# Sink-row products, an opening's marks and a batch of biases placed anew in a fused attention and mixture kernel

## The chip, the cores and the metric

The kernel runs on one core of one Trainium2 chip. The metric is the device time of one execution in microseconds (us). Engines are named PE (TensorE, with PEld for its weight loads), DVE (VectorE), ACT (ScalarE), POOL (GpSimd) and SP (SyncE, which only issues DMAs here).

## The reference, cut to what matters

```python
# 1 attention: batch 4, heads 8, sequence 768, head size 64, n_sink 4, window 128
scores = scale * q @ k.T
keep = (pos_k < n_sink) | ((0 <= pos_q - pos_k) & (pos_q - pos_k < window))
a = exp(where(keep, scores, -1e9) - max);  a /= a.sum(-1) + 1e-9
x = (a @ v) as rows of 512                       # 3072 tokens
# 2 mixture of 8 experts, one expert a token
logits = x @ w_gate + modality_bias[modality_id]
e = argmax(logits);  gate = softmax(logits)[e]
out[e == k] = gate * (relu(x @ w1[k]) @ w2[k])   # 512 -> 1024 -> 512
# 3 dense layer
h = out @ w_in;  g = h * sigmoid(1.702 * h);  return g @ w_out   # 512 -> 2048 -> 512
```

## The kernel before, in words

All three stages lie in one program. Float32 operands of the large products are split into a rounded high part and a low part, and products are added from the parts.

**Attention steps.** Attention runs as 192 steps, 48 for each batch b (step n within it): six query tiles (i = n mod 6) for each of 8 heads. I number them all through as k = 48b + n. In step k PE makes the scores of tile k (L950, L951), turns the probabilities of tile k-3 (`turn_probs`, L964, at i = 5 of that tile also the sink columns, L968) and weighs V with those of tile k-4 (`weigh_values`, L989, L996). DVE masks the scores and finds their minimum (L1802), ACT takes the exponential (L1371), ACT moves turned probabilities out of PSUM (L1406), DVE does so for the sixth tile of a head (L1814, L1815, L1818). Every engine has the same written order, and semaphores bind them: the scores of tile k want the mask of tile k-3 done, for they use three PSUM banks.

**Pairs of heads.** A pair g is two heads, 12 steps. For each pair PE multiplies V transposed by the gate weights and takes the sink rows of V (`weigh_gates`, in two parts, L1016 x6 each and L1022 x2), DVE moves the first (`move_gates`, L1847) and splits the second into a high and a rest (`split_sinks`, L1857, L1859), and ACT lays the split rows out in four blocks (`lay_sinks`, L1398). `ahead(k, at)` says for which pair something falls due in step k. V transposed comes by `load_vt` (L465), issued by SP after it has stored a finished pair (L477) and before it loads further Q, K and V. These loads wait on buffers to come free.

**GpSimd.** POOL splits Q and K of heads 1 to 31 (`split_qk`: L663, L664, L666, L669), and after some heads it does other pieces of work by the dictionary `between`. Head h cannot be scored before its split.

**The opening.** One expert is chosen from batch 0's tokens and two tiles of it are computed while the rest is sorted. POOL adds biases (`open_logits`), marks ties (`open_ties`), counts (`open_chain`, L719), chooses (`open_choice`), makes six one-hot marks (`open_marks`, the marks at L748). DVE does the reductions in between, at fixed steps (`choose_open`, `index_open`), and PE ranks (`rank_open`, step 29 of batch 1) and sorts (`sort_open`, step 17 of batch 2). ACT rounds that expert's weights in 16 pieces at steps given by `cast_at` (L1438), POOL makes their rest in `split_open`.

**The early routing.** The first 18 tiles are routed before attention ends. After its last split POOL adds biases (L788), DVE takes the maximum (L1778, step 34 of batch 3), POOL marks ties (L791 to L795), issues two gathers (`gather_open`, L774) and counts, ending at L817, which sets `tiles_seen`. PE's `rank_early` (L1033) waits for that in step 46 of batch 3 (k = 190), before it turns and weighs.

**After attention** come the opening's products (L1109), the tables and gathers, the runs over experts, and the dense layer.

## Time and profile before

| what | value |
|---|---|
| time, median of 3 runs | 1090.27 us (1090.04 to 1091.02) |
| the profiled execution's own time | 1090.47 us |
| its span, first to last instruction | 1088.7 us |
| mean granted TensorE clock | 0.998 of full |
| busy: PE, PEld, DVE, ACT, POOL | 1077.4, 922.8, 441.6, 405.2, 342.1 us |
| attention, from the first scores to the opening's first product | 10.36 to 222.96 us |

The span leaves 1.8 us of the profiled execution outside of it. A busy PE is a modelled one: ends of matmuls overlap the next ones, so the time of a step is read from start to start, and idle time from the brackets of the timeline. POOL's row in the page is full up to about 217 us and nearly empty afterwards; PE's is full from 10 us to the end.

### The profile page before, as it was taken

The page shows a single profiled execution, that of the slowest core. Times are in us where ns is not written, and L with a number is a line of the kernel's source. Part 1 is how long each engine was busy: PE and PEld are TensorE (multiplying, and loading weights), DVE is VectorE, ACT ScalarE, POOL GpSimd, SP SyncE. Part 2 cuts the span into 40 slices and gives each one's busy share as a digit, 9 for nine tenths or more (in the row PEclk, how much of TensorE's full clock was granted, in tenths as well). Part 3 has the DMA queues.
Part 4 walks back from the last instruction along what each step waited for, and adds up shares of the span by engine and source line. Part 5 has one row for each costly group of instructions (what it writes and reads, how often), then busy time and mean ns, then how long its engine had stood idle before and what let it go on. Part 6 is the DMA issues. An engine that isn't in the chain of part 4 may idle for free.

```text
span 1088.7 us, 18538 instructions
## 1 busy us (share of the span) xinstructions
PE 1077.4 (99%) x5819; PEld 922.8 (85%) x5820; DVE 441.6 (41%) x1137; ACT 405.2 (37%) x863; POOL 342.1 (31%) x425
## 2 busy tenths in 40 slices
PE   9999999999999999999999999999999999999998
PEld 8999999888788888888888888888888888888887
DVE  6777767797122252222463232223323323223222
ACT  5777778743222242222352222222222222222222
POOL 8999999844266221211130010001001001000000
PEclk9999999999999999999999999999999999999999
DMA  9977888253811133121231001001001101000001
GB/s 235 223 178 190 225 222 234 70 176 111 280 41 39 55 129 112 39 87 39 99 116 47 20 20 31 27 0 48 19 10 39 29 10 39 0 0 9 30 1 39
DMA packets 59186, 90.23 MB, mean 83 GB/s; under 512 B 7936, under 2 KB 32512, under 8 KB 59136
## 3 DMA queue, kind: packets, MB, share of 16 engines
q1 hardware_dynamic: 53376, 70.72, 23.5%
q0 software_dynamic: 5760, 18.89, 5.0%
q8 instruction: 25, 0.41, 0.2%
q14 instruction: 25, 0.20, 0.1%
HBM read 70.18 MB, written 19.41 MB: 82 GB/s over the span
## 4 chain that ended last, share of the span: by engine, by line
PE 84%; POOL 9%; DVE 2%; DMA 2%; issue 2%; ACT 1%; POOLq 0%; DVEq 0%; ACTq 0%
PE psum L1295 8%; PE psum L1297 8%; PE psum L1296 8%; PE psum L1288 8%; PE psum L1286 8%; PE psum L1287 8%; PE psum L1226 4%; PE psum L1232 4%; PE psum L1229 4%; PE psum L1195 4%; PE psum L1199 4%; PE psum L989 4%; PE psum L1203 4%; POOL k_lo L669 2%; POOL q_st L666 2%; PE psum L964 2%
## 5 line engine op out<-in xcount | busy, mean ns | idle before, releaser
L2099 DVE TENSOR_TENSOR g<-psum,g 128x512 f32<-128x512 f32 x96 | 66.3, 691 | 292.2 <-ACT g L1535 292.2
L1535 ACT ACTIVATE g<-psum 128x512 f32<-128x512 f32 x96 | 57.4, 599 | 305.3 <-PE psum L1288 304.5
L1295 PE MATMUL psum<-w_hi,gT_hi 128*128 128x512 f32 x384 | 151.3, 394 | 0.0
L1297 PE MATMUL psum<-w_hi,gT_lo 128*128 128x512 f32 x384 | 149.6, 390 | 0.0
L1296 PE MATMUL psum<-w_lo,gT_hi 128*128 128x512 f32 x384 | 149.6, 389 | 0.0
L1288 PE MATMUL psum<-x2T,win_lo 128*128 (+1 forms) x384 | 149.5, 389 | 0.0
L1286 PE MATMUL psum<-x2T,win_hi 128*128 (+1 forms) x384 | 149.5, 389 | 0.0
L1287 PE MATMUL psum<-x2T,win_hi 128*128 (+1 forms) x384 | 149.4, 389 | 0.0
L919 POOL DMA_INDIRECT out<-o_out,out_rows x20 | 21.5, 1076 | 406.2 <-ACT o_out L1555 401.6
L989 PE MATMUL psum<-v_sb,pT 128*128 128x74 f32 x704 | 105.9, 269 | 3.9 <-ACT pT L1406 0.9
L989 PEld LDWEIGHTS psum<-v_sb,pT 128*128 128x128 f32 x704 | 93.9, 192 | 11.4 <-DVE pT L1815 6.5
L1802 DVE CUSTOM_DVE_ANT_0 s_msk<-psum,mask_sb 128x260 f32<-128x260 f32 (+1 forms) x192 | 76.4, 403 | 56.4 <-PE psum L951 39.0
L1371 ACT ACTIVATE probs<-s_msk,negmax 128x260 f32<-128x260 f32 (+1 forms) x192 | 92.7, 494 | 12.2 <-issue 8.3
L2106 DVE TENSOR_TENSOR gT_lo<-g,gT_hi 128x512 fp32r<-128x512 f32 x96 | 66.5, 693 | 64.5 <-ACT gT_hi L1542 64.5
L1542 ACT CAST gT_hi<-g 128x512 fp32r<-128x512 f32 x96 | 59.6, 621 | 74.6 <-DVE g L2099 74.6
L1297 PEld LDWEIGHTS psum<-w_hi,gT_lo 128*128 128x128 f32 x384 | 72.1, 188 | 15.2
L1287 PEld LDWEIGHTS psum<-x2T,win_hi 128*128 128x128 f32 x384 | 72.1, 188 | 15.0
L1288 PEld LDWEIGHTS psum<-x2T,win_lo 128*128 128x128 f32 x384 | 72.1, 188 | 15.0
L1286 PEld LDWEIGHTS psum<-x2T,win_hi 128*128 128x128 f32 x384 | 72.1, 188 | 14.9
L1296 PEld LDWEIGHTS psum<-w_lo,gT_hi 128*128 128x128 f32 x384 | 72.2, 188 | 14.4
L1295 PEld LDWEIGHTS psum<-w_hi,gT_hi 128*128 128x128 f32 x384 | 72.1, 188 | 14.3
L1486 ACT CAST hT_hi<-psum 128x512 fp32r<-128x512 f32 x52 | 28.1, 590 | 120.1 <-PE psum L1214 120.1
(315 smaller groups left out, 1912.8 us busy)
## 6 DMA issues: line engine op xcount, KB each, us to landing
qk_raw<-qkT SPq DMA_DIRECT2D x32, 390.0 KB, 6.3
stage<-w SPq DMA_DIRECT2D x12, 1024.0 KB, 8.6
qk_raw<-qkT SPq DMA_DIRECT2D x32, 198.0 KB, 6.8
x<-y_rows SPq DMA_DIRECT2D x24, 256.5 KB, 2.6
vT_sb<-vT SPq DMA_DIRECT2D x16, 384.0 KB, 4.9
v_sb<-vP SPq DMA_DIRECT2D x16, 384.0 KB, 6.6
x_rows<-x_sb SPq DMA_DIRECT2D x16, 384.0 KB, 3.4
win_raw<-w SPq DMA_DIRECT2D x16, 256.0 KB, 4.5
```

Source lines behind the costliest of these rows:

```text
L989: mm = pe.matmul(o, pT[:, n % 2, k * P:(k + 1) * P], v_sb[:, c, kb, half * VEXT:(half + 1) * VEXT], start=(i == 0 and k == 0), stop=(k == ...
L1286: pe.matmul(bank, wh, hi, start=(c == 0), stop=False)
L1287: pe.matmul(bank, wh, lo, start=False, stop=False)
L1288: mm = pe.matmul(bank, win_lo[:, c, f * P:(f + 1) * P], hi, start=False, stop=(c == CH - 1))
L1295: pe.matmul(psum[:, OB[t], :], gh, hi, start=(f == 0), stop=False)
L1296: pe.matmul(psum[:, OB[t], :], gh, lo, start=False, stop=False)
L1297: return pe.matmul(psum[:, OB[t], :], gT_lo[:, f % 4, t * P:(t + 1) * P], hi, start=False, stop=(f == F2C - 1))
L1371: act.activation(probs[:, n % RING, 0:width[i]], s_msk[:, n % RING, 0:width[i]], ACT.Exp, bias=negmax[:, n % 8:n % 8 + 1], scale=-1.0).the ...
L1542: act.copy(gT_hi[:, f % 4, :], g32[:, f % 2, :]).then_inc(gT_high, 1)
L1802: dve.tensor_tensor_reduce(s_msk[:, n % RING, 0:width[i]], psum[:, S_ps[n % 3], 0:width[i]], mask_sb[:, min(i, MASKS - 1), 0:width[i]], -S ...
L2099: dve.tensor_tensor(g32[:, f % 2, :], psum[:, FB[f % 2], :], g32[:, f % 2, :], ALU.mult)\
L2106: dve.tensor_tensor(gT_lo[:, f % 4, :], g32[:, f % 2, :], gT_hi[:, f % 4, :].bitcast(F32), ALU.subtract).then_inc(gT_split, 1)
```

## The change

The gate products and sink rows of pair g move: pair 0 stays, pair 1 stays, and pair g from 2 on starts in step 3 of pair g-1, where it started in step 9. Spreading is in the same step, the move two steps later, the split three and four later, the laying of one block a step from five to eight later. The six one-hot marks go from POOL to DVE, which compares with an iota row that PE has put into PSUM. POOL's `open_choice` comes after head 15 and no longer 16. The early biases and tie marks, which followed POOL's last split, follow heads 27 and 29. Several of DVE's small steps and PE's two opening products have other step numbers. SP loads V transposed of pair 2 before it loads V of pair 1.

```diff
-    VW_AT, VW_LEAD = 1, 9
+    VW_AT, VW_NEXT, VW_LEAD = 1, 9, 3
-    OPEN_RANK_STEP, OPEN_INV_STEP = 29, 17
+    OPEN_RANK_STEP, OPEN_INV_STEP = 33, 20
+    IOTA_AT = 256
     def ahead(k, at):
-        first, later = k - VW_AT - at, k % (2 * QT) - VW_LEAD - at
-        if first == 0:
-            return 0
-        return k // (2 * QT) + 1 if later == 0 and k // (2 * QT) + 1 < B * PAIRS else None
+        for g in range(B * PAIRS):
+            begin = VW_AT if g == 0 else VW_NEXT if g == 1 else (g - 1) * (2 * QT) + VW_LEAD
+            if k == begin + at:
+                return g
+        return None
...
# SP
             for h in range(SLOT + 1, H):
+                if h == SLOT + 1:
+                    load_vt(2)
                 load_v(0, h - SLOT)
                 sp.wait_ge(qk_split, SPLITS * (h - SLOT))
                 load_qk(0, h)
-                if h == SLOT + 1:
-                    load_vt(2)
...
# GpSimd, open_marks
-                then(pool.tensor_tensor(o_place[:], o_place[:], o_row[:], ALU.add))
+                pool.tensor_tensor(o_place[:], o_place[:], o_row[:], ALU.add).then_inc(open_placed, 1)
...
-                for t in range(QT):
-                    pool.tensor_scalar(open_oh[:, t, :], iota_row[:], o_place[:, t:t + 1], None, ALU.is_equal)\
-                        .then_inc(open_marked, 1)
+                pool.sem_inc(open_placed, 1)
...
+            def add_biases():
+                pool.wait_ge(logits_added, B - 1)
+                pool.tensor_tensor(lg[:, 0:PRE, :], lg[:, 0:PRE, :], bias_of[:, 0:PRE, :], ALU.add).then_inc(biased, 1)
+            def mark_ties():
+                pool.wait_ge(best_found, 1)
...             # the same three operations that stood after the loop
-            between = {2: make_iotas, 5: make_consts, 9: make_biases, 11: open_logits, 12: open_ties, 13: open_chain, 16: open_choice,
-                       18: open_marks, 25: open_rows}
+            between = {2: make_iotas, 5: make_consts, 9: make_biases, 11: open_logits, 12: open_ties, 13: open_chain, 15: open_choice,
+                       18: open_marks, 25: open_rows, 27: add_biases, 29: mark_ties}
...
# PE, weigh_gates
-                    if g == PAIRS + OPEN_RANK_STEP // (2 * QT) + 1:
-                        pe.wait_ge(open_keyed, 1)
                     if g == 2 * PAIRS + OPEN_INV_STEP // (2 * QT) + 1:
-                        pe.wait_ge(open_indexed, 1)
+                        pe.wait_ge(open_marked, QT)
# PE, rank_open
-                pe.wait_ge(vw_moved, 2 * (PAIRS + OPEN_RANK_STEP // (2 * QT) + 1))
-                pe.wait_ge(sinks_split, PAIRS + OPEN_RANK_STEP // (2 * QT) + 1)
+                pe.wait_ge(sinks_split, PAIRS + OPEN_RANK_STEP // (2 * QT) + 2)
...
+                pe.wait_ge(consts_made, 6)
+                pe.matmul(psum[:, VW_ps, IOTA_AT:IOTA_AT + P], ident[:], iota_row[:], start=True, stop=True)
# PE, sort_open
-                pe.wait_ge(vw_moved, 2 * (2 * PAIRS + OPEN_INV_STEP // (2 * QT) + 1))
-                pe.wait_ge(sinks_split, 2 * PAIRS + OPEN_INV_STEP // (2 * QT) + 1)
+                pe.wait_ge(sinks_split, 2 * PAIRS + OPEN_INV_STEP // (2 * QT) + 2)
+                pe.wait_ge(open_placed, 2)
...
# ACT
-                if n < HT and g == 0 and at in (6, 7):
-                    lay_sinks(g, (2 * at - 12, 2 * at - 11))
-                elif n < HT and g and at in (2, 3):
-                    lay_sinks(g, (2 * at - 4, 2 * at - 3))
-                if b == 1 and n == 3 * QT + 2:
+                for t in range(SINK_T):
+                    g = ahead(b * HT + n, 5 + t)
+                    if n < HT and g:
+                        lay_sinks(g, (t,))
+                    if n < HT and g == 0 and t < SINK_T // 2:
+                        lay_sinks(g, (2 * t, 2 * t + 1))
+                if b == 1 and n == 27:
                     act.wait_ge(open_shifted, 1)
...
# DVE, choose_open (batch 1): o_best 12 -> 13, o_lead 18 -> 24, o_gate 22, 23, 24 -> 37, 39, 41,
#   ranks OPEN_RANK_STEP + 1 -> + 2, o_most + 2 -> + 3
-                if n == 18:
+                if n == 24:
                     dve.wait_ge(open_tied, 1)
                     dve.tensor_reduce(o_lead[:], o_tied[:], AX.X, ALU.max).then_inc(open_lead, 1)
...
# DVE, index_open (batch 2)
+                if n in (9, 11, 12):
+                    t = 2 * (9, 11, 12).index(n)
+                    if t == 0:
+                        dve.wait_ge(open_placed, 1)
+                    for t in (t, t + 1):
+                        dve.tensor_scalar(open_oh[:, t, :], psum[:, VW_ps, IOTA_AT:IOTA_AT + P], o_place[:, t:t + 1], None,
+                                          ALU.is_equal).then_inc(open_marked, 1)
-                if n == OPEN_INV_STEP + 2:
+                if n == OPEN_INV_STEP + 3:
...
# DVE, route_early (batch 3)
-                if n == 34:
-                    dve.wait_ge(pre_biased, 1)
+                if n == 25:
+                    dve.wait_ge(biased, 2)
                     dve.tensor_reduce(best[:, pre], lg[:, pre, :], AX.X, ALU.max).then_inc(best_found, 1)
-                if n == 37:
+                if n == 36:
                     dve.wait_ge(ties_marked, 1)
...
-                if n == 44:
+                if n == 45:
                     add_heads(B - 1, H - 2)
# DVE, step
-                if n < HT and at in ((4, 5) if g == 0 else (0, 1)):
-                    split_sinks(g, at % 4)
+                for k in range(2):
+                    if n < HT and ahead(b * HT + n, 3 + k) is not None:
+                        split_sinks(ahead(b * HT + n, 3 + k), k)
```

## Rows read from the trace of the kernel before

**Rows 1.** Busy time by stretch: us, PE, PEld, DVE, ACT, POOL, clock, DMA, GB/s

```profile
74.49:87.20 12.71, 12.59 (x110) 12.26 (x110) 9.24 (x45) 9.90 (x31) 12.13 (x14) 1.00 0.73 186
...
125.58:139.87 14.29, 13.36 (x117) 12.93 (x116) 9.39 (x47) 10.85 (x32) 13.81 (x11) 1.00 0.89 218
139.87:152.82 12.95, 12.75 (x110) 12.25 (x110) 9.07 (x43) 10.70 (x32) 12.63 (x11) 1.00 0.87 219
...
191.90:205.07 13.17, 12.97 (x110) 12.29 (x110) 8.84 (x42) 10.60 (x32) 12.77 (x10) 1.00 0.25 71
205.07:218.21 13.14, 11.64 (x90) 10.19 (x90) 9.29 (x42) 9.96 (x29) 9.07 (x20) 1.00 0.26 71
```

**Rows 2.** Groups of POOL's instructions: count, busy us, mean ns, idle before

```profile
L669 POOL TENSOR_TENSOR k_lo<-qk_raw,k_hi 128x792 fp32r<-128x792 f32 x31 | 58.1, 1874 | 2.4
```

**Rows 3.** The chain that ended last, in order of time: start, us

```profile
120.97 3.51 POOL open_oh L748 x6
...
206.89 0.07 DVE best L1778
```

**Rows 4.** Timeline of POOL: start, us, instruction, idle before

```profile
86.53 0.27 POOL L719 TENSOR_TENSOR o_tied<-o_tied,o_lead 128x48 f32<-128x48 f32 x1
...
124.43 0.82 POOL L663 CAST q_st<-qk_raw 64x768 fp32r<-64x768 f32 x1
...
207.27 0.43 POOL L791 TENSOR_TENSOR below<-lg,best 128x144 f32<-128x144 f32 x1 [0.42 <-DVE best L1778]
...
209.52 1.23 POOL L774 DMA_INDIRECT open_xs<-x_rows,open_gather  x1 [0.57 <-issue]
...
216.39 0.19 POOL L817 CAST seen<-batch_sum 128x8 fp32r<-128x8 f32 x1
```

**Rows 5.** Timeline of PE: start, us, instruction, idle before

```profile
39.44 0.27 PE L964 MATMUL psum<-ident,probs 128*128 128x128 f32 x1
...
49.04 0.31 PE L950 MATMUL psum<-k_hi,q_st 128*128 128x128 f32 x1
...
87.20 0.31 PE L950 MATMUL psum<-k_hi,q_st 128*128 128x128 f32 x1
...
136.01 0.81 PE L1016 MATMUL psum<-sink_w,vT_sb 128*128 128x16 f32 x6 [0.81 <-issue]
...
145.46 0.67 PE L989 MATMUL psum<-v_sb,pT 128*128 128x74 f32 x4
...
217.66 0.23 PE L1033 MATMUL psum<-onehot,tri 128*128 128x144 f32 x1
```

**Rows 6.** Timeline of DVE, the same columns

```profile
49.69 0.29 DVE L1802 CUSTOM_DVE_ANT_0 s_msk<-psum,mask_sb 128x128 f32<-128x128 f32 x1 [0.21 <-ACT probs L1371]
...
49.90 0.36 DVE L1857 TENSOR_SCALAR v_sinks_hi<-psum,signs 128x144 fp32r<-128x144 f32 x1
...
81.36 0.20 DVE L1731 TENSOR_REDUCE o_lead<-o_tied 128x6 f32<-128x48 f32 x1
...
206.89 0.30 DVE L1778 TENSOR_REDUCE best<-lg 128x18 f32<-128x144 f32 x1 [2.08 <-POOL lg L788]
```

**Rows 7.** Timeline of ACT, the same columns

```profile
143.15 0.62 ACT L1438 CAST win_hi<-win_raw 128x512 fp32r<-128x512 f32 x1
...
144.37 0.64 ACT L1398 CAST v_sinks<-v_sinks_all 32x144 fp32r<-32x144 f32 x2
```

**Rows 8.** SP's issue of V transposed for pair 3, and its landing

```profile
35.40 1.57 SPq L465 DMA_DIRECT2D vT_sb<-vT  x1
...
DMA to landing us min/median/max: 4.5/4.5/4.5
```

**Rows 9.** Where the clock fell: one stretch, and PE's timeline in and after it

```profile
246.00:260.00 14.00, 13.98 (x71) 12.01 (x72) 11.02 (x26) 6.23 (x8) 3.28 (x2) 0.88 0.13 39
...
249.21 2.05 PE L1128 MATMUL psum<-win_hi,hT_hi 128*128 128x512 f32 x4
...
259.34 1.18 PE L1128 MATMUL psum<-win_hi,hT_hi 128*128 128x512 f32 x4
```

More of the change, by code:

```diff
@@ L378, in program @@
         spare_known = sem("spare_known")
-        logits_added, pre_biased, best_found = sem("logits_added"), sem("pre_biased"), sem("best_found")
+        logits_added, biased, best_found = sem("logits_added"), sem("biased"), sem("best_found")
         ties_marked, lead_found = sem("ties_marked"), sem("lead_found")
         expert_known, consts_copied = sem("expert_known"), sem("consts_copied")
-        open_biased, open_best, open_shifted, open_tied = (sem(f"open_{k}") for k in ("biased", "best", "shifted", "tied"))
+        open_best, open_shifted, open_tied = (sem(f"open_{k}") for k in ("best", "shifted", "tied"))
         open_lead, open_exped, open_gated, open_seen = (sem(f"open_{k}") for k in ("lead", "exped", "gated", "seen"))
         open_ranked, open_keyed, open_chosen = (sem(f"open_{k}") for k in ("ranked", "keyed", "chosen"))
-        open_expert_known, open_marked, open_inverted = (sem(f"open_{k}") for k in ("expert_known", "marked", "inverted"))
+        open_expert_known, open_placed, open_marked = (sem(f"open_{k}") for k in ("expert_known", "placed", "marked"))
+        open_inverted = sem("open_inverted")
         open_indexed, open_high, open_split, open_low = (sem(f"open_{k}") for k in ("indexed", "high", "split", "low"))
@@ L776, in gather_open @@
                         .then_inc(open_gathered[t], 16)
-            between = {2: make_iotas, 5: make_consts, 9: make_biases, 11: open_logits, 12: open_ties, 13: open_chain, 16: open_choice,
-                       18: open_marks, 25: open_rows}
+            def add_biases():
[3 more added lines that the diff above has]
+                pool.wait_ge(best_found, 1)
+                pool.tensor_tensor(below[:, 0:PRE, :], lg[:, 0:PRE, :], col(best[:, 0:PRE], some), ALU.subtract)\
+                    .then_inc(shifted, 1)
+                pool.wait_ge(shifted, 1)
+                then(pool.tensor_scalar(tied[:, 0:PRE, :], below[:, 0:PRE, :], 0.0, None, ALU.is_equal))
+                pool.tensor_tensor(tied[:, 0:PRE, :], tied[:, 0:PRE, :],
+                                   from_end[:].rearrange("p (o e) -> p o e", o=1).broadcast_to(some), ALU.mult)\
+                    .then_inc(ties_marked, 1)
+            between = {2: make_iotas, 5: make_consts, 9: make_biases, 11: open_logits, 12: open_ties, 13: open_chain, 15: open_choice,
+                       18: open_marks, 25: open_rows, 27: add_biases, 29: mark_ties}
             for h in range(1, B * H):
@@ L785, in _ @@
                     split_open(h - OPEN_BACK)
-            pool.wait_ge(logits_added, B - 1)
-            pool.tensor_tensor(lg[:, 0:PRE, :], lg[:, 0:PRE, :], bias_of[:, 0:PRE, :], ALU.add).then_inc(pre_biased, 1)
-            pool.wait_ge(best_found, 1)
-            pool.tensor_tensor(below[:, 0:PRE, :], lg[:, 0:PRE, :], col(best[:, 0:PRE], some), ALU.subtract)\
-                .then_inc(shifted, 1)
-            pool.wait_ge(shifted, 1)
-            then(pool.tensor_scalar(tied[:, 0:PRE, :], below[:, 0:PRE, :], 0.0, None, ALU.is_equal))
-            pool.tensor_tensor(tied[:, 0:PRE, :], tied[:, 0:PRE, :],
-                               from_end[:].rearrange("p (o e) -> p o e", o=1).broadcast_to(some), ALU.mult)\
-                .then_inc(ties_marked, 1)
             gather_open()
@@ L1725, in choose_open @@
                 counts = psum[:, VW_ps, OPEN_RANK + QT * E:OPEN_RANK + (QT + 1) * E]
[L1726 to L1727 removed]
+                if n == 13:
+                    dve.wait_ge(biased, 1)
                     dve.tensor_reduce(o_best[:], o_lg[:], AX.X, ALU.max).then_inc(open_best, 1)
[L1729 removed]
+                if n == 24:
                     dve.wait_ge(open_tied, 1)
                     dve.tensor_reduce(o_lead[:], o_tied[:], AX.X, ALU.max).then_inc(open_lead, 1)
[L1732 removed]
+                if n == 37:
                     dve.wait_ge(open_exped, 1)
                     then(dve.tensor_reduce(o_gate[:], o_exps[:], AX.X, ALU.add))
[L1735 removed]
+                if n == 39:
                     then(dve.tensor_scalar(o_gate[:], o_gate[:], 1e-9, None, ALU.add))
[L1737 removed]
+                if n == 41:
                     dve.reciprocal(o_gate[:], o_gate[:]).then_inc(open_gated, 1)
[L1739 removed]
+                if n == OPEN_RANK_STEP + 2:
                     dve.wait_ge(open_ranked, 1)
```

15 lines of the change are left out of this document (3 added, 12 removed).

## The prediction

> **What bounds the kernel now.** I read the page first: PE is full from 10 us to the end, POOL up to 217 us, so all that this edit touches lies in attention. The chain of waits then shows who leads there. From 120.97 us on, POOL's marks and its splits stand in it, up to DVE's maximum at 206.89 [rows 3]; the reader should not take this for a PE that waits on splits. POOL is never short of work: 31 splits of 5.4 us each, of which one of four instructions is shown, have 2.4 us of idle before them in all [rows 2]. But PE starts each head 2 to 7 us after its split. What makes the chain run along POOL is that its early biases stand behind the last split, and DVE stops 2.08 us for them in step 34 [rows 6], which stops PE.
>
> Stretches of one pair, from scores to scores, give PE's own pace: 12.71 us where nothing disturbs [rows 1]. Above that I find: 1.58 us in 125.58:139.87; 0.24 in 139.87:152.82 and likewise in the two pairs behind it; 0.46 in 191.90:205.07 and in the pair ahead of it; and 205.07:218.21, which is the last pair's first eleven steps. Those should take 12.71 less one step (0.9) and less the gate products that it does without (1.5), 10.3, and take 13.14 [rows 1].
>
> The point that decides is the last wait. PE's ranking product starts at 217.66 [rows 5]; it needs POOL's last count, which ends at 216.39 + 0.19 = 216.58 [rows 4]. PE reaches that place only 1.1 us after POOL is ready. So of what PE gains, only 1.1 us count before POOL must gain as well. The end of attention, the opening's products and the long rest hang on this point, and I carry a shift of it unchanged to the end.
>
> **PE's side, part by part.**
> - Gate products of pair g from step 9 to step 3. PE's count of work is the same. In a head without them PE waits in its fourth step for DVE's move of the sixth tile (some 0.3 us); the products cover that wait. Covered heads and bare heads change places, 14 for 14. Nothing.
> - The old wait for the index. Products of pair 10 (k = 117) waited for DVE: 0.81 us idle [rows 5], 1.05 in the step. They now lie at k = 111 and wait only for marks that DVE ends in k = 108. Gain 1.05. The remaining 0.53 of the 1.58 is the sort, which moves to k = 116 and stays.
> - ACT. In even heads two blocks, one rounded weight piece (0.62) and two more blocks (0.64 for two) pile up [rows 7], and PE's product at 145.46 [rows 5] comes 0.24 late. With one block a step in the odd head the heap is 1.24 us by the step that was late, where it was 1.9. I take all of it as gone: 6 x 0.24 + 3 x 0.21 = 2.1, with 0 as the other end.
> - DVE's stop for the biases. Of the 2.8 us that the last stretch has above its pace, 0.2 are the ranking and 0.45 ACT's heap; 2.1 are left, as long as DVE's wait of 2.08 [rows 6]. I take 1.9, for PE may run on a little. Gone, for POOL adds them after head 27, at about 181 us, and DVE asks at k = 169, about 191.
> - The ranking of the opening moves from k = 77, where it cost 0.2, to the bare fourth step of k = 81, where PE would wait anyway; the added iota product (0.2 by the spacing of two 128-column products) goes there too. Gain 0.2 to a loss of 0.2; I take 0.1.
> - Six marks on DVE. No row has this form from PSUM. Nearest: a 128x144 scaling out of PSUM takes 0.36 [rows 6]; so at most 6 x 0.36 = 2.2 us in three steps, at least 0 for PE, as DVE has 0.8 us idle in the fourth step and 0.4 in the sixth. I take 0.2.
> - V transposed of pair 3. This is a new wait. It was wanted at k = 33, about 45 us; now at k = 27. It is issued at 35.40 and lands 4.5 later, at 39.9 [rows 8], and SP cannot be earlier, as its queue is jammed by the store ahead. PE comes to k = 27's products at 39.44 [rows 5], where ahead of that it turned probabilities. So PE stands 0.5 us. For other pairs the load lands 2 us or more ahead. Bounds: 0, and 1.5 if the earlier stores shift. ACT's spreading waits with it, 0.3 us of work that PE's second part does not miss. The swap of pair 2's load and pair 1's V on SP costs nothing: both land by about 24, wanted at 26 and 28.
>
> Sum for PE: 1.05 + 2.1 + 1.9 + 0.1 - 0.2 - 0.5 = 4.4; it would come to the ranking at about 213.2.
>
> **POOL's side.** Its last count at 216.58 shifts by:
> - marks removed: from 120.97 [rows 3] to 124.43 [rows 4], -3.46.
> - a new wait after head 13. `open_chain` starts at 86.53 [rows 4], and now DVE gives the lead in k = 72, not in k = 66. PE starts k = 72 at 87.20 [rows 5]. Mask follows scores by 0.65 (49.04 [rows 5] to 49.69 [rows 6]), the next operation starts 0.21 behind, and the reduction takes 0.20 (81.36) [rows 6]: 87.20 + 0.65 + 0.21 + 0.20 = 88.26, with 0.1 for the semaphore 88.35. That is 1.8, and as PE is 0.5 late by pair 3's load, 2.3. Behind the waiting instruction stand the splits of heads 14 on; those have 3 us and more to spare, so PE misses nothing, but every later piece of POOL is late by it. Lower end 1.8, upper 3.3.
> - choice after head 15: POOL is there at 102.6, DVE's key is ready at 101.3. No wait.
> - biases and ties moved ahead of the last splits. Before, from 206.37, the end of the last split, to the gathers at 209.52 [rows 4] it is 3.15 us, 0.42 of it the wait for the maximum. After: biases 0.43 and ties 1.63 among splits, and 0.61 from the last split to the gathers: 2.67. So -0.48. The splits of heads 30 and 31 end at about 201.9 and 207.3; PE wants them at 202.5 and 208.5.
>
> Sum: -3.46 + 2.3 - 0.48 = -1.6. The last count ends at 216.58 - 1.6 = 215.0, PE ranks at 215.1, 1.9 us after it came there. The kernel is 217.66 - 215.1 = 2.6 us shorter. Behind the wait PE's products stand close, so I give nothing back there.
>
> Span 1088.7 - 2.6 = 1086.1; the profiled execution 1090.47 - 2.6 = 1087.9. That execution lies 0.2 above the median of 1090.27, which gives 1087.7. All that PE gains beyond POOL is lost in that wait; so even if ACT's heap stays (2.1), the time barely moves.
>
> **Rivals.**
> - PE is the bound (chance 0.13). If POOL's new wait is absent or its counting has slack, PE comes at 213.2: 4.4 shorter, 1085.9; if pair 3's load does not stop it, 1085.4. For it speaks that the range of both sums overlaps within a microsecond or so; against it, that DVE cannot give the lead before scores of k = 72 exist.
> - No change to be measured (0.17). POOL waits longer, by 2 us more in all: 1088.5 to 1090.3. A PE that is late in any step up to k = 72 passes its lateness to POOL one for one, so a load of pair 3 that lands at 41.5 would do the most of it. For: SP's issue of that load took 1.57 us, where others take 0.5. Against: SP's order from 16 us on is the same as before.
> - The clock (0.10). PE's new stop of 1.9 us comes in a stretch of small products. In the old trace the clock is 0.88 over 246 to 260 [rows 9], that is, at 1.2 GHz for a part and 2.4 for the rest, after small transposes and 64-column products; four 512-column products took 2.05 instead of 1.18 there [rows 9], and with the next four 1.5 us were lost. The stops of 0.5 to 0.8 us in attention cost no clock. If the new one does, 1.5 us are given back: 1089.2. [...]
> - Slower (0.10). The bare fourth step. If the products in step 3 do not cover the even head's wait while the odd head's is bared, and ACT's rounding with blocks in the same steps adds its 0.24, PE loses 0.3 + 0.24 in each of 14 pairs, 7.6 us, against gains of 4.4: PE ranks at 220.8, 3.1 later, 1093.4. It decides from 0.3 us a pair on, and can be told from 0.5. Against it: DVE does the same in-head steps in both heads, and old odd heads with products show no wait.
>
> **Chances and range.** The forecast, 1086.9 to 1088.8, has 0.50. A tell-tale difference from no change is 0.2%, 2.2 us, so faster begins below 1088.1: two thirds or so of the forecast and all of the first rival make 0.48, and same is 0.42; slower 0.10. For eight in ten I take 1085.3 to 1090.5, which holds all but the slow case and some of the tails.
>
> **What would show it.** In the changed trace: POOL idle about 2.3 us before L719's successor, on DVE's lead; PE idle about 0.5 us at pair 3's products near 39.5 and about 1.9 us before the ranking near 213; no idle at k = 117; DVE's maximum with no wait; pairs of 12.7 us from 140 to 200. If PE is not idle before the ranking, POOL is not the bound, and the second sum holds. Wrong would be the forecast if a pair's pace is no longer 12.71, or if the long rest behind 223 us does not shift as one piece.

## The result and the profile after

The changed kernel takes 1099.01 us, the median of 6 runs (1097.22 to 1103.53), beside 1090.28 (1090.04 to 1091.54) for the kernel before: a ratio of 1.0089, 95% interval 1.0075 to 1.0103. It is 8.7 us slower. The forecast was 1087.7 us, with 0.10 for slower.

The profiled execution took 1097.22 us, its span 1095.5. PE's first scores start at 9.96 us in it (10.36 before). Two marks carry the comparison: POOL's last count, and PE's ranking product, which follows it. From the timeline of the changed kernel (start us, us, engine, line):

```profile
224.35 0.19 POOL L822 CAST seen<-batch_sum 128x8 fp32r<-128x8 f32 x1
...
226.65 0.23 PE L1036 MATMUL psum<-onehot,tri 128*128 128x144 f32 x1
```

Before, the count ended at 216.58 [rows 4] and PE ranked at 217.66 [rows 5]. So the ranking is 9.0 us later, and it comes 2.1 us after the count is done: PE, not POOL, is late. At the end of the span 6.7 of the 9.0 are left. Most of the difference is a part of 246 to 260 us that the old profiled execution had at 1.2 GHz (it cost 1.5 us, by the spacing of PE's products there); the same window of the changed kernel has a granted clock of 1.00. Stretches from scores to scores, in the columns of [rows 1]:

```profile
63.58:77.89 14.31, 13.32 (x110) 12.36 (x110) 9.87 (x44) 10.00 (x30) 13.76 (x12) 1.00 0.71 174
77.89:91.37 13.48, 13.13 (x111) 12.37 (x110) 9.24 (x44) 9.98 (x30) 8.40 (x9) 1.00 0.69 175
132.98:147.20 14.22, 13.95 (x117) 13.07 (x116) 10.16 (x47) 11.02 (x32) 13.82 (x13) 1.00 0.80 202
147.20:160.68 13.48, 13.12 (x111) 12.35 (x110) 9.41 (x47) 11.03 (x32) 13.16 (x11) 1.00 0.81 211
202.02:215.59 13.57, 13.21 (x110) 12.36 (x110) 9.26 (x44) 10.88 (x32) 10.37 (x11) 1.00 0.23 70
215.59:227.21 11.62, 11.21 (x91) 10.13 (x90) 8.86 (x40) 9.56 (x28) 7.50 (x16) 1.00 0.26 80
```

The reader should see three things. An undisturbed pair takes 13.48 us and not 12.71 [rows 1], with the same count of instructions on PE (111 and 110 in the stretch) and a full clock: PE waits. The pair at the start of a batch takes 14.31 (three of them do, k = 48, 96 and 144). And what the change meant to remove did go: the last stretch, to PE's ranking step, takes 11.62 where it was 13.14.

Who is waited for stands in the view of waits (us in total, times, longest). The changed kernel:

```profile
PEld psum L994 <- ACT pT L1410: 12.7, 35, 0.8
POOL o_tied L721 <- DVE o_lead L1736: 5.8, 1, 5.8
POOL below L786 <- DVE best L1789: 5.1, 1, 5.1
```

and the same wait of PE's weight loads in the kernel before:

```profile
PEld psum L989 <- ACT pT L1406: 3.8, 11, 0.8
```

POOL's two waits of 5.8 and 5.1 us look like the culprit in such a list. They are not: PE's ranking does not follow POOL by the shortest step, as the first fence shows. The new waits are PE's on ACT's move of turned probabilities, 35 where there were 11. The timeline of PE shows their spacing at the start of an even head, by the first score product (L955) of k = 84, 85 and 86 in the changed kernel:

```profile
91.37 0.31 PE L955 MATMUL psum<-k_hi,q_st 128*128 128x128 f32 x1
...
92.64 0.37 PE L955 MATMUL psum<-k_hi,q_st 128*128 128x260 f32 x1
...
93.90 0.36 PE L955 MATMUL psum<-k_hi,q_st 128*128 128x260 f32 x1
```

Each of these steps takes 1.27 us, where they take 0.86 and 0.91 before. And ACT in that stretch, where it lays the blocks that stand in steps k = 82 and 83 of its written order:

```profile
91.41 0.31 ACT L1402 CAST v_sinks<-v_sinks_all 32x144 fp32r<-32x144 f32 x1
91.74 0.37 ACT L1410 COPY pT<-psum 128x256 f32<-128x256 f32 x1
92.14 0.51 ACT L1375 ACTIVATE probs<-s_msk,negmax 128x260 f32<-128x260 f32 x1
92.68 0.31 ACT L1402 CAST v_sinks<-v_sinks_all 32x144 fp32r<-32x144 f32 x1
93.01 0.37 ACT L1410 COPY pT<-psum 128x256 f32<-128x256 f32 x1
```

From move to move it is 1.27 us (91.74 to 93.01), ACT never idle: move, exponential and one block, one behind the other. The kernel before, where no block lay between, in the timeline of ACT:

```profile
79.41 0.37 ACT L1406 COPY pT<-psum 128x256 f32<-128x256 f32 x1
79.81 0.51 ACT L1371 ACTIVATE probs<-s_msk,negmax 128x260 f32<-128x260 f32 x1
80.23 0.35 ACT L1406 COPY pT<-psum 128x256 f32<-128x256 f32 x1
80.48 0.51 ACT L1371 ACTIVATE probs<-s_msk,negmax 128x260 f32<-128x260 f32 x1
81.00 0.37 ACT L1406 COPY pT<-psum 128x256 f32<-128x256 f32 x1
```

There a move starts before the exponential ahead of it has ended (80.23 against 79.81 + 0.51), and from move to move it is 0.77 to 0.82 us. A block of 0.31 us thus lengthens this chain by 0.45 or more, and the step of PE beside it has only 0.1 us to spare.

The batch starts have a second cause. VectorE's timeline at n = 6 and 7 of batch 2 (k = 102 and 103) in the changed kernel:

```profile
127.53 0.36 DVE L1868 TENSOR_SCALAR v_sinks_hi<-psum,signs 128x144 fp32r<-128x144 f32 x1
127.92 0.84 DVE L1665 TENSOR_REDUCE lg<-lg_parts 128x48 f32<-128x384 f32 x1
129.09 0.43 DVE L1813 CUSTOM_DVE_ANT_0 s_msk<-psum,mask_sb 128x260 f32<-128x260 f32 x1 [0.33 <-ACT probs L1375]
```

The sum over the heads of the batch before (`add_heads` at n = 6) now stands behind the first half of V's split, which used to lie elsewhere in a pair, and the mask of k = 103 starts at 129.09, 1.5 us behind PE's scores of that step (127.54). PE pays for it two steps on: k = 57, 105 and 153 take 1.96 to 1.98 us instead of 1.41. That is 0.55 of the 0.83 us that such a pair takes above 13.48; the other 0.29 lie at k = 50, 98 and 146 (1.36 us, where the same step of a later pair takes 1.07). At k = 50 and 146 most of them go when ACT's blocks are placed otherwise (1.05 to 1.12 us in the runs below).

### The profile page after: what moved, and what is told of

It reads as the page before. It is cut to its first block, busy times and chain, and to the rows that moved or that the text cites. A ratio compares the mean times of both kernels' runs of the same rounds, so it can differ in the third digit from the quotient of the medians.

```text
span 1095.5 us, 18568 instructions
## 1 busy us (share of the span) xinstructions
PE 1081.7 (99%) x5821; PEld 922.4 (84%) x5822; DVE 444.1 (41%) x1143; ACT 407.8 (37%) x863; POOL 340.4 (31%) x419
## 4 chain that ended last, share of the span: by engine, by line
PE 89%; ACT 4%; issue 2%; DVE 2%; DMA 2%; POOL 1%; POOLq 0%; DVEq 0%; ACTq 0%
PE psum L1299 8%; PE psum L1301 8%; PE psum L1300 8%; PE psum L1292 8%; PE psum L1290 8%; PE psum L1291 8%; PE psum L994 5%; PE psum L1230 4%; PE psum L1236 4%; PE psum L1233 4%; PE psum L1199 4%; PE psum L1203 3%; PE psum L1207 3%; PE psum L969 2%; PE psum L1218 2%
## 5 line engine op out<-in xcount | busy, mean ns | idle before, releaser
L994 PE MATMUL psum<-v_sb,pT 128*128 128x74 f32 x704 | 109.0, 274 | 8.2 <-DVE pT L1826 2.6
```

The lines of the kernel that those rows point to most:

```text
L994: mm = pe.matmul(o, pT[:, n % 2, k * P:(k + 1) * P], v_sb[:, c, kb, half * VEXT:(half + 1) * VEXT], start=(i == 0 and k == 0), stop=(k == ...
```

## The experiments

All comparisons are with runs of the kernel before made beside them. To set profiled executions side by side I use the distance from PE's first scores to its ranking: 207.3 us before (217.66 - 10.36) and 216.7 after (226.65 - 9.96), so 9.4 us is what has to be explained. Where a profiled execution has a stretch at half clock inside that distance, I take out what its steps took above the same steps of a neighbouring kernel, and say so.

**Two blocks a step in the quiet steps.**

```diff
-                for t in range(SINK_T):
-                    g = ahead(b * HT + n, 5 + t)
-                    if n < HT and g:
-                        lay_sinks(g, (t,))
+                for t in range(SINK_T // 2):
+                    g = ahead(b * HT + n, 5 + t)
+                    if n < HT and g is not None:
+                        lay_sinks(g, (2 * t, 2 * t + 1))
```

> The changed kernel with one thing put back: ScalarE lays two blocks a step, in the third and fourth step of the odd head (k = 8, 9 mod 12), not one a step in k = 8 to 11. Theory (ScalarE is the bound in a pair since a block lies in steps 4 and 5 of a head, where it also moves probabilities in every step): a pair of batch 1 or 2 goes from 13.48 back to 12.7 us, 14 to 15 pairs give 11 us back at PE's ranking (226.65 to about 215.5), and the kernel takes 1087 to 1090 instead of 1099.0. Rival (the gate products in the even head's fourth step, or V's split on VectorE in steps 6 and 7, slow the pair): the pair stays at 13.3 us or more, the time at 1097 or more. Each pair that crosses the start of a batch keeps its extra 0.8 us by both.

Measured: 1091.16 us (12 runs), before 1091.19 (29), ratio 1.0012 (0.9995 to 1.0030). A pair, in the view of stretches of this kernel:

```profile
50.70:63.42 12.72, 12.60 (x110) 12.27 (x110) 9.04 (x42) 9.87 (x31) 12.05 (x13) 1.00 0.80 199
```

The ranking comes 209.4 us after the first scores, 207.2 without the 2.3 us that k = 9 to 12 took too long in this one execution: 0.7 in k = 9, where PE stood for the load of pair 1's V transposed (landed at 19.75 us, in the other profiled kernels between 17.6 and 18.4), the rest at half clock from 22.4 us on. That is 9.5 us less than 216.7, all of the 9.4, and the main theory holds: ACT's blocks are the loss. I had put the time at 1087 to 1090, and the median came out 1.2 us above; part of what was missing is in the later pairs, where two blocks and a rounded weight piece share a step (k = 83 and 107 take 1.40 us, not 0.95, and k = 131 and 143 take 1.26).

**One block a step, in quiet steps only.** The four blocks at k = 8, 9, 14 and 15 mod 12:

```diff
+                for t, late in enumerate((5, 6, 11, 12)):
+                    g = ahead(b * HT + n, late)
+                    if n < HT and g is not None and g > 1:
+                        lay_sinks(g, (t,))
```

> The changed kernel with one block a step, but only in ScalarE's two quiet steps of each head: k = 8, 9, 14, 15 mod 12 instead of 8 to 11. Theory (it is the place of a block, not the number in a step): as with two blocks a step in k = 8 and 9, a pair of 12.7 us and 1087 to 1090 us, within 1 us of that kernel. Rival (one block a step is slow by itself, as each starts ScalarE's chain anew): a pair between 12.9 and 13.5, over 1092.

Measured: 1088.99 us (12 runs), before 1091.19, ratio 0.9983 (0.9967 to 0.9998). The undisturbed pairs fall to 12.65 us, under the 12.71 of the kernel before (pairs 0 and 1 keep two blocks a step). The ranking comes 210.05 us after the first scores, 204.9 without the 5.1 us that k = 27 to 32 took too long (see pair 3 below), 11.7 less than in the changed kernel:

```profile
79.13:91.78 12.65, 12.53 (x110) 12.26 (x110) 9.25 (x44) 9.99 (x31) 7.78 (x8) 1.00 0.73 187
```

One block a step is no harm in itself; the place is.

**The blocks alone, in the kernel before.**

```diff
-                elif n < HT and g and at in (2, 3):
-                    lay_sinks(g, (2 * at - 4, 2 * at - 3))
+                elif n < HT and g and at in (2, 3, 4, 5):
+                    lay_sinks(g, (at - 2,))
```

> The kernel before with one thing of the change: blocks of V's sink rows are laid one a step, in k = 2, 3, 4, 5 mod 12 of the even head, not two a step in k = 2 and 3. All else, gate products and splits too, stays. Theory (a block in steps 4 and 5 makes ScalarE the bound): 0.6 to 0.8 us more a pair, 15 pairs, so 9 to 12 us: 1099 to 1102. Rival (the loss of the change needs the moved products or splits): within 2 us of 1090.3.

Measured: 1098.43 us (6 runs), before 1091.19, ratio 1.0072 (1.0055 to 1.0090). The ranking is 216.6 us after the first scores, 9.3 later than before. Its pairs:

```profile
77.74:91.21 13.47, 13.11 (x110) 12.33 (x110) 9.23 (x45) 10.14 (x31) 12.12 (x20) 1.00 0.72 183
```

One edit of the change, alone, gives its undisturbed pair of 13.47 to 13.48 us and as large a loss at the ranking. The sums agree partly by chance: each of the two kernels has losses and gains of its own in single steps (here k = 75 takes 2.56 us instead of 1.42, and the stop for the biases at k = 181 to 183, 1.75 us, is hidden). The moved gate products are not needed for the slow pair, and with ACT's blocks out of the way they do not slow it either (12.72 and 12.65 us above).

**Half the dose.** One block in the last two steps of a head, where the change has two:

```diff
+                for late, blocks_of in ((5, (0, 1)), (6, (2,)), (7, (3,))):
+                    g = ahead(b * HT + n, late)
+                    if n < HT and g:
+                        lay_sinks(g, blocks_of)
```

> The changed kernel with blocks at k = 8 (two), 9 (one) and 10 (one) mod 12: one block in the head's last two steps, where there were two. Theory (ScalarE has no room in these steps, so each block there is lateness in full and is worked off in the next head's first steps): half of the loss, 0.4 us a pair: a pair of 13.1 us, PE's ranking 211.9 us after its first scores (207.1 with both blocks out of these steps, 216.7 with both in them), time 1093 to 1094.5. Rival (there is a point beyond which the pair tips over): a pair of 12.7 or of 13.5 us, the time within 1.5 us of one of the two.

Measured: 1093.83 us (5 runs), before 1089.19 (17 runs), ratio 1.0042 (1.0026 to 1.0057); the ranking 210.5 us after the first scores, 1.4 less than I had put. A pair:

```profile
76.26:89.31 13.05, 12.79 (x110) 12.28 (x110) 9.22 (x44) 9.86 (x30) 9.81 (x9) 1.00 0.69 175
```

A pair takes 12.65, 13.05 and 13.48 us with none, one and two blocks in those steps: 0.40 and 0.43 each. There is no tipping point between none and two; each such block costs one step of 1.27 us at the start of the next head, where 0.86 or 0.91 is the pace.

**The sum over the heads two steps later.** On top of two blocks a step:

```diff
-                if b and n == PV_LAG + 2:
+                if b and n == PV_LAG + 4:
                     add_heads(b - 1, H)
```

> Two blocks a step as in the first kernel of this call, and the sum over the heads of the batch before (VectorE, 0.64 us) two steps later in a batch, at n = 8 instead of n = 6, where V's split now stands. Theory (the sum and the split in one step make the 0.55 us by which k = 57, 105 and 153 are late): these steps fall to 1.4 us, 1.6 us less in all at PE's ranking; 1 to 1.6 us less than with two blocks a step alone where PE leads, nothing where GpSimd does. Rival (the stretch is late by something else): k = 57, 105, 153 stay at 1.9 us and the time is the same within 0.3 us.

Measured: 1089.48 us (12 runs), before 1091.19, ratio 0.9990 (0.9977 to 1.0004). The steps k = 57, 105 and 153 take 1.41 or 1.42 us, as expected, and the ranking is 205.9 us after the first scores, 1.3 less than with two blocks alone.

**Both places put right.** One block in each quiet step and the sum at n = 8; then the same with the opening's lead at n = 18, as before:

```diff
-                if n == 24:
+                if n == 18:
                     dve.wait_ge(open_tied, 1)
```

> One block in each quiet step (k = 8, 9, 14, 15 mod 12) and the sum over the heads at n = 8 of a batch. Theory (both losses of the change are places: ScalarE's blocks, and VectorE's sum beside V's split): k = 57, 105 and 153 fall from 1.95 to 1.4 us, PE's ranking comes 1.6 us sooner after PE's first scores than with the blocks alone (203.3 against 204.95 without the time at half clock, 207.3 before), and the kernel takes 1.0 to 1.6 us less than that one: 1086.5 to 1088 beside 1090.3 to 1091.2 before. Rival (GpSimd, which waits for VectorE's lead up to 93.2 us, now ends its counting after PE is there): at most 0.6 us less, and PE idle ahead of its ranking.

> The same, and the opening's lead on VectorE at n = 18 of batch 1 as in the kernel before, not n = 24. Theory (PE is the bound; GpSimd's wait of 5.4 us ahead of its chain is hidden): GpSimd's chain starts at 88 and not 93 us, and the time stays within 0.5 us of the kernel with n = 24. Rival (GpSimd is the bound by now): PE's ranking and the time come 0.5 to 2 us sooner.

Measured: 1088.20 and 1087.83 us (12 runs each), before 1090.10 (35), ratios 0.9992 (0.9980 to 1.0004) and 0.9992 (0.9976 to 1.0007). These say less than the profiles. With the lead at n = 24, POOL's count ends at 214.75 us and PE ranks at 214.90, 204.6 us after its first scores and not 203.3. So short a step from POOL to PE looks like a wait for POOL, but PE's timeline shows none:

```profile
214.66 0.28 PE L955 MATMUL psum<-k_hi,q_st 128*128 128x260 f32 x1
...
214.90 0.30 PE L1036 MATMUL psum<-onehot,tri 128*128 128x144 f32 x1
```

The ranking stands 0.24 us behind the scores of k = 190, as in the kernel before (217.66 - 217.42), and that step takes 0.86 us, where it takes 0.80 in the kernel before and 0.79 with the lead at n = 18: POOL can have cost 0.07 us at most. The missing 1.3 us lie in PE's own steps: 0.34 at k = 27 (pair 3, below), and 0.87 in steps behind the new place of the sum over the heads, 0.12 each at k = 62 and 158 and 0.63 at k = 109 and 110 (1.01 and 1.55 us, instead of 0.91 and 1.02), just behind VectorE's marks at k = 105, 107 and 108. With the marks on POOL (a run below) k = 109 and 110 take 0.91 and 1.14, so 0.5 us of this are the marks. With the lead at n = 18 POOL's chain starts at 86.99 us, not 88.82, and the count is done 0.35 us before PE ranks, 205.4 us after its first scores; k = 27 took 2.85 us in that execution, 0.87 more than in the other, and without it the two rankings lie within 0.1 us. So of the first expectation neither the 203.3 nor its rival (PE idle ahead of its ranking) came; of the second, that PE is the bound holds.

**Pair 3's V transposed.** At k = 27 the products of pair 3 wait for a load. In the timeline of PE of the kernel with one block in each quiet step:

```profile
38.42 0.28 PE L956 MATMUL psum<-k_lo,q_st 128*128 128x260 f32 x1
40.41 0.81 PE L1019 MATMUL psum<-sink_w,vT_sb 128*128 128x16 f32 x6 [1.70 <-issue]
```

and shortly behind, in its view of stretches (granted clock in the third column from the end, 0.50 of 2.4 GHz, that is 1.2 GHz):

```profile
42.40:49.20 6.80, 6.80 (x35) 6.79 (x34) 3.44 (x16) 3.50 (x11) 6.64 (x5) 0.50 1.04 278
```

In the eight profiled kernels that want this load at k = 27, the load lands between 39.5 and 41.8 us, and k = 27 takes 1.64 us (no wait; three of them, the changed kernel among these), 1.83, 1.98, 2.85, 3.58 and 4.04. In the two longest PE had stood 1.70 and 2.15 us, and both then fell to 1.2 GHz (at 42.4 and 44.6 us); in the kernel shown here k = 27 to 32 took 5.1 us too long, standing included. Where k = 27 took 2.85 us PE had stood 0.97 us, and the clock stayed at 2.4 GHz until 239.9 us. The changed kernel is spared because ACT's loss brings PE to the step later, at 40.24, when its load has landed at 39.87. One run puts pair 3's products alone back to their old place, with that pair's blocks two a step from k = 38:

```diff
+            if g == 3:
+                begin = 2 * (2 * QT) + 9
```

> One block in each quiet step, the sum at n = 8, the lead at n = 18, and the gate products of pair 3 alone at their old place (from k = 33; blocks of that pair two a step from k = 38), so that its V transposed is wanted 4 us later. All else of the change stays. Theory (the wait that the prediction put at 0.5 us is 0.2 to 2.2 us from one execution to the next, and in the longer ones the clock falls behind it): k = 27 takes 1.41 us in the profile, and the executions with a clock under 0.997 become as rare as with the kernel before; the median falls by about 1 us, to 1086.5 to 1087 beside 1090 before, and the mean by more. Rival (the stop at k = 27 costs nothing at the end, and clock dips come anywhere): the median within 0.5 us of that of the kernel without this edit, 2.3 us under the one before, and as many executions under 0.997.

Measured: 1085.82 us (5 runs, 1084.65 to 1085.94), before 1090.11 (9), ratio 0.9960 (0.9946 to 0.9974). k = 27 takes 1.40 us; all five executions have a granted clock of 0.998 or more, where 4 of the 12 without this edit had 0.996 or less (five are few: by chance alone none of the four would fall among them about one time in five). The ranking is 204.3 us after the first scores, with POOL 0.36 us ahead of it:

```profile
213.72 0.19 POOL L824 CAST seen<-batch_sum 128x8 fp32r<-128x8 f32 x1
...
214.27 0.23 PE L1038 MATMUL psum<-onehot,tri 128*128 128x144 f32 x1
```

So the change with three places altered (blocks, sum, pair 3) and its lead put back is 4.3 us faster than the kernel before. Of these, 3.0 lie ahead of the ranking; the profiled execution has no stretch at half clock either, where that of the kernel before has one behind its ranking [rows 9].

**Biases among the splits, alone.** In the kernel before:

```diff
-                       18: open_marks, 25: open_rows}
+                       18: open_marks, 25: open_rows, 27: add_biases, 29: mark_ties}
...
-                if n == 34:
+                if n == 25:
```

> The kernel before with one thing of the change: biases and ties of the first three batches on GpSimd after heads 27 and 29, VectorE's maximum and lead at n = 25 and 36, and its sum over six heads at n = 45. Theory of the prediction (GpSimd's last count holds PE's ranking, 1.1 us behind PE's own pace): VectorE's stop of 2.08 us goes, but the count comes only 0.5 us sooner, PE ranks 206.8 us after its first scores (207.3 before) and the kernel is 0.5 us shorter. Rival (GpSimd's counting only follows VectorE's lead, and PE sets the end): 1.6 to 2.2 us shorter.

Measured: 1088.52 us (11 runs), before 1090.10, ratio 0.9983 (0.9974 to 0.9991). The timeline of POOL and PE:

```profile
215.60 0.19 POOL L822 CAST seen<-batch_sum 128x8 fp32r<-128x8 f32 x1
...
215.94 0.30 PE L1038 MATMUL psum<-onehot,tri 128*128 128x144 f32 x1
```

From the first scores (10.03) the count ends at 205.76 us, 0.46 sooner than before (216.58 - 10.36 = 206.22), just what the prediction had (0.48). The ranking is 1.4 us sooner, and here my expectation was wrong in its arithmetic, not in its mechanism: it left out the 1.08 us by which PE used to come behind the count. 0.46 and 1.08, less the 0.15 that PE still lies behind, are the 1.4. Here PE is held: k = 190 takes 1.13 us, where it takes 0.80 in the kernel before. The time fell by 1.6 us, which is the lower end of the rival's range; but the rival had PE set the end, and these rows show POOL doing it by 0.3 us.

**VectorE's marks, alone.** In the kernel before, two each at n = 11, 12 and 14 of batch 2, since PE writes that bank of PSUM at other steps there:

```diff
+                if n in (11, 12, 14):
+                    t = 2 * (11, 12, 14).index(n)
...
+                        dve.tensor_scalar(open_oh[:, t, :], psum[:, VW_ps, IOTA_AT:IOTA_AT + P], o_place[:, t:t + 1], None,
+                                          ALU.is_equal).then_inc(open_marked, 1)
```

> The kernel before with one thing of the change: VectorE makes the opening's six marks out of PSUM, two each at n = 11, 12 and 14 of batch 2, GpSimd makes none. Theory of the prediction: GpSimd's later work is 3.46 us earlier, its biases are ready before VectorE asks in step 34 (2.08 us of wait gone), and the marks cost PE 0.2: PE's ranking 1.7 us sooner, 205.6 us after its first scores, the kernel 1.7 us shorter. Rival (marks out of PSUM at 0.2 to 0.36 us each stop PE in full three steps): 0.4 us or more lost in each of k = 107, 108 and 110, and the kernel at most 0.7 us shorter.

Measured: 1088.89 us (11 runs), before 1090.10, ratio 0.9985 (0.9976 to 0.9994). The ranking is 207.6 us after the first scores; 1.55 of that are k = 118 to 120 at half clock, so 206.0: 1.3 sooner. The marks themselves stop PE nowhere in k = 107, 108 or 110; 0.12 us show up at k = 111 (and 0.16 at k = 159, a batch later, unexplained), and 0.23 at k = 77, where PE now makes the iota product. My 1.7 was 0.4 too high.

**All but VectorE's marks.** One block in each quiet step, sum at n = 8, lead at n = 18, marks on POOL:

```diff
+                for t in range(QT):
+                    pool.tensor_scalar(open_oh[:, t, :], iota_row[:], o_place[:, t:t + 1], None, ALU.is_equal)\
+                        .then_inc(open_marked, 1)
```

> One block in each quiet step, the sum at n = 8, the lead at n = 18, and the opening's six marks back on GpSimd, with no iota product on PE: all of the change but VectorE's marks. Theory (the marks on VectorE cost PE more than they give now that biases stand among the splits): k = 109 and 110, which took 1.01 and 1.55 us with marks on VectorE, take 0.91 and 1.02, k = 81 0.2 less, and the kernel 0.5 to 1.0 us less than with them, 1086.8 to 1087.3 beside 1090.1 before. Rival (GpSimd, 3.5 us later by its marks, holds the ranking): the same or up to 1.5 us more.

Measured: 1095.79 us (6 runs), before 1089.19, ratio 1.0051 (1.0031 to 1.0070). My theory fell, and its rival was too mild. The waits of PE from 190 to 223 us:

```profile
PE psum L1037 <- issue: 2.1, 1, 2.1
PE psum L958 <- POOL k_lo L671: 0.9, 2, 0.6
```

PE waits for POOL's splits at k = 168 and 180 and for its count (L1037 is the ranking; the count ends at 221.54 and PE starts at 221.69). With biases ahead of the last splits, POOL's marks push those splits past their time, which they did not before. This profiled execution had also stood 2.15 us at k = 27, and its PE was late from there on, so the sizes of these waits are not those of the marks alone. But all six executions are slow: the fastest, 1091.51 us at a granted clock of 0.998, lies 2.4 to 4.7 us above the five of the kernel with VectorE's marks at that clock. VectorE's marks are what makes room for the biases. The stop ahead of the ranking also has a price behind it: PE stands 2.15 us up to 221.69, and from 222.1 to 225.5 us its clock is at 1.2 GHz:

```profile
222.20:225.40 3.20, 3.20 (x18) 3.20 (x17) 1.17 (x5) 1.99 (x6) 0.00 (x0) 0.50 0.00 0
```

**Built from the kernel before.** Products and splits where they were; biases among the splits; marks on VectorE; ACT's blocks at k = 3 and 8 mod 12, two each:

```diff
-                elif n < HT and g and at in (2, 3):
-                    lay_sinks(g, (2 * at - 4, 2 * at - 3))
+                elif n < HT and g and at in (3, 8):
+                    lay_sinks(g, (0, 1) if at == 3 else (2, 3))
```

> The kernel before, with its gate products and splits where they were, plus three things: biases and ties among GpSimd's splits, marks by VectorE out of PSUM, and ScalarE's four blocks two at k = 3 and two at k = 8 mod 12, apart from the rounded weight piece's heap. Theory: PE loses neither VectorE's stop (1.6 us) nor ScalarE's heap (0.24 us in six pairs, 0.21 in three), and GpSimd's counting is 3.9 us sooner, so it does not hold PE: PE's ranking 204.0 us after its first scores (207.3 before), the time 3.3 us less than before: 1086.8. Rival (heap and stop are hidden behind GpSimd's counting, or VectorE's marks take the gain): 1.5 us less, as each part alone gave, 1088.5.

> The kernel ahead of this one in the call, with the opening's sort one step sooner in batch 2 (k = 112, not 113), so that VectorE's index is ready sooner for the products of pair 10 at k = 117. Theory: of the 1.05 us that k = 117 takes too long, 0.8 or more go, k = 117 takes at most 1.9 us where it took 2.69, and the time is 0.8 us less, 1086.0. Rival (the wait moves to the sort or to VectorE's next step): the pair's start to start stays at 14.3 us.

Measured: 1085.93 us (12 runs) and 1085.46 us (5 runs), before 1089.19 (17), ratios 0.9974 (0.9962 to 0.9986) and 0.9961 (0.9946 to 0.9975). The rankings are 203.9 and 202.9 us after the first scores, where 204.0 and 0.8 less were expected. The stretch with the opening's sort, without and with the sort one step sooner:

```profile
126.06:140.47 14.41, 13.38 (x117) 12.95 (x116) 10.76 (x53) 10.98 (x32) 14.01 (x13) 1.00 0.94 234
```

```profile
125.65:139.08 13.43, 13.19 (x117) 12.93 (x116) 10.77 (x53) 10.87 (x32) 13.11 (x12) 1.00 0.88 226
```

Both kernels of this part beat both kernels of the case; against the one with pair 3 put right (1085.82 beside 1090.11) the ratios 0.9961 and 0.9960 do not tell a winner.

## Why the prediction was wrong

**The step that failed is the term "ACT" of PE's side.** It said: "With one block a step in the odd head the heap is 1.24 us by the step that was late, where it was 1.9. I take all of it as gone", a gain of 2.1 us with 0 as the other end. The blocks cost 9.3 us instead by that edit alone in the kernel before, and their undoing in the changed one gives 9.5 us back, or 11.7 with one block in each quiet step. So the step that failed is a wait put at nothing: PE's on ACT's moves in the steps that received the blocks. The term counted how much work lay in the step that used to be late, and never asked what ACT does in the steps the work went to. Without a block ACT goes from move to move in 0.77 to 0.82 us, and the steps of PE beside which the blocks of steps 4 and 5 are laid (k = 84 and 85 above) take 0.86 and 0.91; four blocks in quiet steps could be worked off, a block in steps 4 or 5 could not. Its bound "0 as the other end" was no bound for a move into other steps. The rival "bare fourth step" had named 0.54 us a pair and the time 1093.4, but put the cause at the products and ACT's rounding; neither was it. The prediction's own sign of being wrong, a pair whose pace is no longer 12.71 us, did come.

**The sum over the heads** was missing altogether. The prediction counted the split's move as free for VectorE and did not look at which other work of VectorE stands at n = 6 and 7 once in a batch. It costs 0.55 us three times.

**What held.** The stop for the biases goes: the last stretch is 13.14 before [rows 1] and 10.86 with two blocks a step; k = 181 to 183 give back 1.75 us, for 1.9. The index wait: k = 116 and 117 take 0.74 us above their pace, where k = 113 and 117 took 1.59 above it, a gain of 0.85 for 1.05. Moving the gate products: nothing, 12.65 to 12.72 us a pair. Marks: 0.35 at k = 77 and 111 by the run with them alone, for 0.2; with the sum at n = 8 just ahead of them, 0.5. POOL's new wait for the lead is 2.19 us with ACT's blocks and the sum put right, for 2.3 (5.8 in the changed kernel, whose PE and VectorE are late). The sum on POOL's side, -1.6: in that same kernel the count is 204.41 us after the first scores, -1.8.

**What of the last wait.** That POOL's count can hold PE's ranking is shown, by 0.3 us with the biases alone and by 2.15 us with the marks on POOL. The wait of 1.9 us that was to set the time is not: no profiled version of the change with VectorE's marks has it. PE ranks at 214.90 us with the lead at n = 24, where the prediction had 215.1, but it comes there by its own pace, so that this number fits is luck. PE's side was put at 4.4 us, the stop for pair 3 (0.5) included. With blocks, sum and pair 3 put right, and so without that stop, PE ranks only 3.0 us sooner than before. Some 1.8 us of what is missing are in steps that the prediction did not have: 0.87 behind the new place of the sum over the heads, 0.32 at k = 87, 0.41 at k = 98 and 0.20 at k = 93.

**V transposed of pair 3** was named as a wait (0.5 us, bounds 0 and 1.5). It is 0 in the changed kernel, for a bad reason, 0 in two more and 0.2 to 2.4 us in the other five. The prediction took its size from one execution, and one landing time is not a bound.

**The clock rival** had the right coupling. Its stop ahead of the ranking did not come in the changed kernel; where one of 2.15 us did come, with the marks on POOL, the clock fell within a microsecond (222.1 to 225.5 us). The Trainium skill, "TensorE: Matmul & The Clock Gate", section "HAM oscillation — how this bites in real kernels", ties waits on DMA, longer ones than these and repeated in a loop, to a fall of PE's clock; the trace agrees in kind at k = 27, with a single wait of 1.70 us and 42.4 to 49.2 us at 0.50. It is not a full account: kernels here fell at other places too. Before, it is 249 us, with no stop of 0.5 us or more near it; in the run with marks alone it is 138.6, 2.8 us behind a stop of 0.81 us that the kernel before and two more have without a fall.

Small terms that I had not seen lie in the second batch and just behind it, where the change moves VectorE's steps of the opening: k = 93 takes 1.61 us, 0.2 above its pace, in each profiled version of the change, and with one block in each quiet step k = 87 and 98 take 0.3 and 0.4 more (k = 98 with two blocks a step too). They were not tried one by one, and their cause stays open.

## What to carry to other kernels

When work is spread out to shorten a heap, write down for every step that receives it what the engine does there and what the step's pace is: four blocks in two steps with slack were free, two of them in steps with 0.1 us of slack cost 0.83 us a pair. A total of busy time does not show it, for ACT was busy 74% of such a pair. Before a wait on a load is moved forward, look at the load's landing in several executions; a term of 0.5 us there cost up to 2.4, and the clock behind it more.

The Trainium skill, "Perfetto Trace Analysis", section "Optimizing Scalar/DVE Operations", says that breaking up instructions may let work end sooner where an engine is not saturated but makes others wait. The four blocks are four instructions in every version here, and what helped was not how many a step got but which steps: two a step and one a step in quiet places gave pairs of 12.72 and 12.65 us, one a step across k = 8 to 11 mod 12 gave 13.48.

## What the runs showed of the hardware

- A block of 0.31 us on ScalarE made its chain from move to move 0.45 to 0.50 us longer (1.27 us, where it was 0.77 to 0.82): without it a move out of PSUM starts 0.09 us before the exponential ahead of it ends, with it each instruction starts after the one ahead. The busy time of the instruction was not its price in this chain.
- The same load, of 384 KB, wanted at the same step in eight kernels, landed between 39.5 and 41.8 us, 4.0 to 6.0 us after its issue.
- TensorE's clock fell to 1.2 GHz at different places in executions of nearly the same kernel (22.4 to 25.8 us, 42.4 to 49.2, 44.6 to 48, 138.6 to 142, 222.1 to 225.5, 249 to 252), and those up to 142 us cost 1.6 to 3.2 us each, the stop ahead of them not counted. Two of them followed stops of 1.70 and 2.15 us on a load, one a stop of 0.47 us, and one a stop of 2.15 us on POOL's count; a stop of 0.97 us was followed by none in attention. Single executions of kernels that differ by 1 us can't be ranked without looking at the granted clock first.
- VectorE's marks out of PSUM, two in a step that has room, did not stop PE in any of their three steps in the kernel before; with the sum over the heads at n = 8, just ahead of them, they made k = 109 and 110 0.5 us longer.
